# An attention, expert and MLP kernel on one core: two VectorE instructions swapped, a GpSimd step and sixteen transposes moved

## What is computed

```python
# 1. attention with a decaying complex state: B=4, H=8, S=768, D=48
mag = sqrt(a_re**2 + a_im**2); scale = minimum(mag, 0.999) / (mag + 1e-6)
for t in range(S):
    new_re = ar * S_re - ai * S_im          # ar, ai: a_re, a_im times scale at step t
    new_im = ar * S_im + ai * S_re
    S_re, S_im = new_re + outer(k[t], v[t]), new_im
    y[t] = q[t] @ S_re
# 2. x = y as 3072 rows of 384; each row goes to the one of 8 experts with the highest logit
h = relu(xe @ w1[e]); out[mask] = gate_w * (h @ w2[e])
# 3. h = (x @ m1) * (x @ m2) @ m3; result = h @ m_out
```

## Time and profile before

| | |
|---|---|
| median of 3 runs | 1012.51 us (1010.46 to 1018.81) |
| the profiled execution | 1015.03 us |
| its span, first to last instruction | 1013.3 us |
| TensorE busy | 924.8 us (91%) |
| VectorE busy | 439.8 us (43%) |
| ScalarE busy | 412.1 us (41%) |
| GpSimd busy | 394.7 us (39%) |
| mean granted TensorE clock | 0.980 |

### The profile page before, as it was taken

How to read it: one execution, slowest core, us unless ns; L and a number is a source line. 1 busy time by engine, 2 the same in 40 slices (tenths; PEclk the granted TensorE clock), 3 DMA queues, 4 the chain that set the end, 5 groups by cost and what they waited for, 6 DMA issues and landing times.

```text
span 1013.3 us, 17941 instructions
## 1 busy us (share of the span) xinstructions
PE 924.8 (91%) x6799; PEld 818.8 (81%) x6799; DVE 439.8 (43%) x703; ACT 412.1 (41%) x620; POOL 394.7 (39%) x230
## 2 busy tenths in 40 slices
PE   1678999889889699989999999998999999999996
PEld 1568888778878466979999999997898989898986
DVE  2559889979967360252222222222313131313130
ACT  4768798688654232232322322321222222222221
POOL 6336476676745342573373657610010101010101
PEclk9779999999999999999999999999999999999999
DMA  7714434534365147541532553411010101000000
GB/s 200 137 33 95 87 72 79 126 79 81 78 186 189 41 176 234 172 136 61 164 112 101 165 172 103 166 40 48 1 63 1 63 1 63 1 32 1 32 1 32
DMA packets 160151, 91.81 MB, mean 91 GB/s; under 512 B 128576, under 2 KB 152896, under 8 KB 160064
## 3 DMA queue, kind: packets, MB, share of 16 engines
q1 hardware_dynamic: 147344, 67.81, 25.1%
q10 hardware_dynamic: 9648, 13.30, 4.2%
q0 software_dynamic: 3072, 9.49, 2.4%
HBM read 71.77 MB, written 18.81 MB: 89 GB/s over the span
## 4 chain that ended last, share of the span: by engine, by line
PE 71%; DVE 15%; POOL 5%; issue 5%; ACT 2%; another core or an unknown queue 1%; DMA 0%; SPq 0%; ACTq 0%; DVEq 0%; POOLq 0%
PE psum L1840 19%; PE psum L1799 13%; PE psum L1777 12%; PE psum L1852 10%; PE psum L401 6%; PE psum L1686 4%; PE psum L1623 2%; DVE arena L1182 2%; DVE arena L1114 2%; DVE arena L1133 1%; PE psum L1649 1%; POOL x_by_expert L690 1%; DVE arena L1121 1%; POOL arena L671 1%; POOL arena L659 1%
## 5 line engine op out<-in xcount | busy, mean ns | idle before, releaser
L1840 PE MATMUL psum<-x2t,ring 128*128 128x512 f32 x864 | 197.1, 389 | 0.0
L1840 PEld LDWEIGHTS psum<-x2t,ring 128*128 128x128 f32 x864 | 162.1, 188 | 33.5
L401 PE MATMUL psum<-arena 128*128 128x128 f32 x925 | 130.3, 283 | 38.3 <-DVE arena L1114 21.9
L401 PEld LDWEIGHTS psum<-arena 128*128 128x128 f32 x925 | 110.2, 146 | 53.7 <-issue 42.8
L784 POOL DMA_INDIRECT out_dram<-arena x24 | 23.1, 963 | 320.9 <-ACT arena L1093 317.4
L1777 PE MATMUL psum<-ring,f_xt 128*128 x558 | 137.2, 400 | 4.4 <-DVE f_xt L1474 4.4
L1799 PE MATMUL psum<-ring,f_ht 128*128 x744 | 138.7, 341 | 2.0 <-DVE f_ht L1480 2.0
L1799 PEld LDWEIGHTS psum<-ring,f_ht 128*128 128x128 f32 x744 | 129.7, 190 | 2.4 <-issue 2.3
L1777 PEld LDWEIGHTS psum<-ring,f_xt 128*128 128x128 f32 x558 | 103.7, 190 | 26.0 <-issue 4.9
L1515 DVE TENSOR_TENSOR ab_f<-psum,a_sb 128x512 f32<-128x512 f32 x48 | 33.2, 692 | 204.6 <-ACT a_sb L1083 204.6
L1852 PE MATMUL psum<-wfold_half,ab 128*128 128x384 f32 x576 | 102.8, 336 | 0.0
(11 more groups left out here) (178 smaller groups left out, 1371.1 us busy)
## 6 DMA issues: line engine op xcount, KB each, us to landing
stage<-in_moe_w_dram SPq DMA_DIRECT2D x16, 1536.0 KB, 7.3
y_dense<-arena ACTq DMA_DIRECT2D x31, 194.0 KB, 2.7
arena<-x_by_expert ACTq DMA_DIRECT2D x28, 194.0 KB, 2.4
arena<-y_dense SPq DMA_DIRECT2D x24, 194.0 KB, 3.6
arena<-in_a_re_dram SPq DMA_DIRECT2D x24, 192.0 KB
arena<-in_a_im_dram SPq DMA_DIRECT2D x24, 192.0 KB
arena<-in_q_dram SPq DMA_DIRECT2D x24, 192.0 KB, 2.7
arena<-in_k_dram SPq DMA_DIRECT2D x24, 192.0 KB, 3.4
```

The lines of the kernel that those rows point to most:

```text
L401: return nc.tensor.transpose(psum[:, bank, c0:c0 + P], src, ident)
L1840: last = mm(psum[:, bank + j % 2, :], m_half[m][x][:, kc, j * P:(j + 1) * P], x2t[y][:, kc, :], start=(kc == 0 and x + y == 0), stop=(kc = ...
```

## The change

On VectorE, `clip(p)` goes ahead of `unit_check(p)`, and `ratio(p)` moves from ahead of the masks to behind the state. On GpSimd, `sum_angles` of a unit moves from the end of a unit's last step (i = 2, unit n + 2) into the next step (i = 0, unit n + 1), behind the three `root_prod` and ahead of the second half of the row sends and of `turn_q`. On TensorE and ScalarE, the transposes of fold blocks 2 and 3 and their copies move ahead of the last batch's ranks and exponential; the transposes now wait for the last masks, since they write the banks of the scores. Where the transposes stood, the count is followed by the first fold.

```diff
--- before.py
+++ after.py
@@ -698,7 +698,7 @@
 
             def step(k):
                 n, i = divmod(k, K)
-                p = n + 2
+                m, p = n + 1, n + 2
                 if i == 1 and k >= PICKED + 1 and (k - PICKED - 1) % C == 0:
                     tag_rows((k - PICKED - 1) // C)
                 if i == 2 and k >= PICKED + 2 and (k - PICKED - 2) % C == 0:
@@ -706,6 +706,8 @@
                 if i == 0 and 0 <= n < U:
                     for x in range(K):
                         root_prod(n, x)
+                if i == 0 and 0 <= m < U:
+                    sum_angles(m)
                 if i == 0 and k >= PICKED + 3 and (k - PICKED - 3) % C == 0:
                     scatter_rows((k - PICKED - 3) // C, K, C)
                 if 0 <= k < K * U:
@@ -714,8 +716,6 @@
                     add_squares(p)
                 if i == 1 and 0 < p < U:
                     ratio_seed(p)
-                if i == 2 and 0 <= p < U:
-                    sum_angles(p)
 
             add_squares(0)
             ratio_seed(0)
@@ -981,6 +981,8 @@
             for k in range(-4, K * U + 1):
                 step(k)
             rows_out(NT - 1)
+            fold_cols(EARLY, m3t_late)
+            fold_cols(EARLY + 1, m3t_late)
             exp_logits(B - 1)
             act.wait_ge(bad_ready, 1)
             with act.If(act.value_load(bad[0:1, 0:1], min_val=0, max_val=1) > 0):
@@ -998,9 +1000,8 @@
                     nc.scalar.activation(ex, lg, ACT.Exp).then_inc(g_exp, 1)
 
 
-            fold_cols(EARLY, m3t_late)
             for i in range(EARLY, NJ):
-                if i + 1 < NJ:
+                if EARLY < i < NJ - 1:
                     fold_cols(i + 1, m3t_late)
                 if i == EARLY:
                     act.wait_ge(y_done, K * U)
@@ -1303,8 +1304,6 @@
                         ends((a - 1) // K)
                 if i == 2 and k >= PICKED + 2 and (k - PICKED - 2) % C == 0:
                     weigh((k - PICKED - 2) // C)
-                if i == 2 and 0 < p < U:
-                    ratio(p)
                 if k == -1:
                     fold_cols(0, m3t_early)
                     fold_cols(1, m3t_early)
@@ -1312,6 +1311,8 @@
                     mask(k - 1)
                 if k >= 2 and (k - 2) % C < C - 1:
                     state(k - 2)
+                if i == 2 and 0 < p < U:
+                    ratio(p)
                 if 0 <= k < K * U:
                     weigh_inputs(n, i)
                     turn_k(n, i)
@@ -1322,8 +1323,8 @@
                 if i == 0 and k >= PICKED and (k - PICKED) % C == 0:
                     pick((k - PICKED) // C)
                 if i == 1 and 0 < p < U:
+                    clip(p)
                     unit_check(p)
-                    clip(p)
                 if i == 2 and 0 <= m < U:
                     inverse(m)
                 if k == 0:
@@ -1673,6 +1674,8 @@
                 for half in range(2):
                     if i:
                         pe.wait_ge(m3t_copied, 2 * i - 1 + half)
+                    if i == EARLY and half == 0:
+                        pe.wait_ge(att_masked, 2 * K * U)
                     for j in range(4):
                         last = tr(A_BANK + half, j * P, m3s[m3_buf(i)][:, (4 * half + j) * P:(4 * half + j + 1) * P])
                     last.then_inc(m3t_done, 1)
@@ -1722,6 +1725,8 @@
             for k in range(-4, K * U + 1):
                 step(k)
             rows_t(NT - 1)
+            fold_t(EARLY, m3_late)
+            fold_t(EARLY + 1, m3_late)
             rank_rows(B - 1, rank_done, hot_done)
             pe.wait_ge(bad_ready, 1)
             with pe.If(pe.value_load(bad[0:1, 0:1], min_val=0, max_val=1) > 0):
@@ -1744,11 +1749,10 @@
             mm(psum[:, RANK_BANK, COUNT_COL:COUNT_COL + E], ones, seen, start=True, stop=True).then_inc(count_done, 1)
 
             pe.wait_ge(x_done, NT)
-            fold_t(EARLY, m3_late)
-            for i in range(EARLY, NJ):
-                if i + 1 < NJ:
+            for i in range(EARLY, NJ - 1):
+                if i > EARLY:
                     fold_t(i + 1, m3_late)
-                    fold(i, m3t_late, mo_late)
+                fold(i, m3t_late, mo_late)
 
             pe.wait_ge(table_ready, 1)
```

## The result

| | before | changed |
|---|---|---|
| median | 1012.54 us (20 runs, 1008.92 to 1018.81) | 1015.86 us (20 runs, 1013.64 to 1017.92) |
| ratio, 95% interval | | 1.0035 [1.0023, 1.0047] |
| profiled execution | 1015.03 us, span 1013.3 | 1016.47 us, span 1014.8 |
| mean granted TensorE clock | 0.980 | 0.979 |

The changed kernel is 3.3 us slower. The forecast was 1014.7 us, range 1004 to 1019, within 1% at 0.88: it held. Several terms under it did not. The prediction took 10 us for the least that can be told of this kernel; twenty runs of each told 3.3. The profile of before lies 2.5 us above its median, the one of after 0.6 above its own, so their difference of 1.4 us is smaller than the 3.3 of the medians. I compare the traces step by step instead. A step is named by the chunk whose scores TensorE computes in it.

A forecast was written before the change was run, and what follows sets the result against it. TensorE, 71% of the chain, was taken to bound the kernel, with VectorE's chain to `turn_k` inside each unit. Terms 0.6 - 0.3 + 2.5 + 0.5 + 0.8 - 1.9 = +2.2 us gave a median of 1014.7, range 1004 to 1019.

The forecast's parts named there:

- The copy L1138 is held: VectorE's 12-element copy inside SBUF waits until GpSimd's L636 ends, about 2 us instead of 0.16.
- rival (a): The copy L1138 does not wait, so `turn_k` comes 1.4 us earlier in ordinary units; sum -6.1, 1006.4 us; chance 0.20.
- Clip, six units: VectorE's stall moves from L1114 to L1138, `turn_k` gains 0.06 us a unit; -0.3 us over six units, bounds -7 and 0.
- Prologue: Same edit for unit 1: L1138 waits, so the copies that let TensorE start the first fold start later; +0.6 us.
- step 0: Unit 1's two sums now stand between root products and `turn_q`; TensorE's wait grows from 2.95 to near 5.4; +2.5 us.
- nothing hides it: At the first step's `turn_q`, the reason for taking the upper of the bounds 0 and 2.5 us as the delay.
- Sums, ordinary units: `turn_q` comes 0.4 us later with 0.5 to spare; VectorE's 0.95 gained in the inverse lies beside TensorE's work; 0 us.
- the units in which the expert is picked: Two units bound by VectorE: the pick is still held by GpSimd's add of squares, 0.4 us later; +0.8 for two.
- Sums, units that send rows: Two units where TensorE waits for GpSimd's L671: 0.4 us later less 0.1 from earlier sends; +0.5 for two.
- Transposes: Tail: 16 transposes move into TensorE's idle time, 3.4 us gone, 1.6 lost to the first fold at half speed; -1.9 us.
- the upper bound: In the tail: +4.0 us if loads of blocks 6 and 7, about 8 us earlier, delay TensorE's code behind the branch.
- Rival (b): `turn_q` of a unit's first chunk, behind GpSimd between inverse and scores, bounds every unit; +4 on top, 1018.7 us; chance 0.12.

The follow-up runs named there:

- e4_ends_late: Changed kernel with the 12-column copy of the ends moved behind the state; 1003.87 us against 1009.52 for the kernel before, ratio 0.9938.
- e5_sum1_early: Changed kernel with unit 1's sums of angles back in the prologue; one run for its trace: step 0 scores 9.8 us after the inverse's start, 12.4 in the changed kernel.
- e2_sums: Kernel before with only the sums of angles moved; 1012.78 us against 1009.52, ratio 1.0036.
- e1_clip: Kernel before with only the clip ahead of the sum check and the ratio behind the state; 1009.63 us against 1009.52, ratio 0.9995.
- e10_best: Kernel before with clip first, ratio and copy of the ends behind the state, transposes moved, block 6 and 7 loads held until the count; 1004.09 us against 1013.63, 0.9898.
- e11_after_filler: Changed kernel with 24 constant transposes ahead of the scores of steps 12 and 18; 1013.71 us against 1013.63 for the kernel before, 0.9991; changed kernel beside it 1015.69.
- e8_sums_filler: Kernel before with only the sums moved, plus 24 constant transposes ahead of the scores of steps 12 and 18; 1012.84 us against 1008.0 for the kernel before, 1.0041.
- e3_transposes: Kernel before with only the transposes and their copies moved; 1009.34 us against 1009.52, ratio 0.9993.
- e6_loads_late: Changed kernel with SyncE holding the loads of m3 blocks 6 and 7 until the count; one run for its trace: the wait ahead of the count 3.38 us.
- e7_clip_ends: Kernel before with clip first, ratio and copy of the ends behind the state, sums and transposes as before; 1001.37 us against 1008.0, ratio 0.9938.

## Why the prediction was right, point by point

- **The copy L1138 is held: right.** 2.25 us beside L636, in eight places 1.98 in the mean. On the rule of the Trainium skill that the prediction cites, SBUF — State Buffer, "Who interferes with whom", the trace now agrees: the copy, second to issue, waited until GpSimd's instruction ended. This was the step on which "same" and not "faster" hung, and e4_ends_late shows it: with the copy elsewhere the gain of rival (a) is there. Rival (a) stood 8.3 us below the forecast (1006.4 for 1014.7); taking the copy away brought 6 to 10 us.
- **Clip, six units: -0.3 forecast.** In the unit shown it is -0.2 (10.04 to 9.82), near -1.3 if all six gain as much.
- **Prologue +0.6 and step 0 +2.5: together 3.1 forecast, +0.34 measured at step 1.** In the prologue the delay of the copies was right (L1212 starts 6.1 us after L1111, 5.6 before), but nothing of it is left at the inverse (22.8 us after L1111, 22.9 before). At step 0 the delay of the scores was right (12.4 for 9.85), the step "nothing hides it" failed, and the wait ahead of the scores, forecast near 5.4, is 0.28: TensorE had run these scores at half clock, and now the phases, waiting for the sums too, ran directly ahead of them and took the low clock on themselves. That the profile before had lost the clock there is chance (e5_sum1_early); in an execution that kept it, the step would have been right.
- **Sums, ordinary units: 0 forecast**, right at steps 6 and 21, **-0.93 measured** at step 3. There the inverse's shorter second half (2.71 to 1.76) lies on VectorE's chain to the next `turn_k`; I had put it beside TensorE's work. (L1149 fell to 1.76 in seven of its eight places, at the last it is 2.72.) In the units in which the expert is picked I forecast +0.4 each; they gained 0.93 and gave back 0.8.
- **Sums, units that send rows: +0.5 forecast, +5.4 measured.** This is the mis-sized term that makes the kernel slower, and e2_sums carries the whole loss. Steps 12 and 18 lose 1.46 and 1.16. Of that, the sums ahead of the sends and `turn_q` cost 0.6 each, twice what was counted. At step 12 another 0.87 comes from the first half of the inverse, held by L671; this is not the doing of the moved sums, since in e1_clip and e10_best, where they are in their old place, L671 held it too (it took 3.90 us, 1.05 later from inverse to scores). At step 18 the other 0.55 stands ahead of the inverse. Steps 13 and 19 then lose 1.25 and 1.51 to the clock, which I had put at nothing; e11_after_filler got about 2 of the two back, e8_sums_filler did not.
- **Transposes: -1.9 forecast, +0.6 between the two profiles, about -1 in the mean of six traces with and six without, nothing that the timing of e3_transposes can tell.** 3.4 us left, as counted. The first fold cost 2.8 more in place of 1.6, as it ran some 5.5 us at 0.50. And of the upper bound, a longer wait ahead of the count, some 1.2 us came true, which e6_loads_late took away again; that it is a wait for code remains a guess.

The sum of the terms by these traces is 0.3 - 1.3 - 0.9 - 0.3 + 5.4 + 0.6 = +3.8 against +2.96 found at block 4; the rest of -0.8 lies mostly between step 23 and `rows_t`. That the forecast's +2.2 came near the +3.3 of the medians is luck in the sizes: a loss of 5 us that I did not see stood against gains that I did not see, and against delays that were hidden. The mechanism of the clip was right; the one that makes the kernel slower, the clock behind the sends, is not in the prediction. Rival (b) had the place right, GpSimd between inverse and scores, and at step 12 also its condition, an inverse held by another GpSimd instruction. It did not come true in the ordinary units (12.8 us from inverse to scores at step 6, as before), and its 4 us came near only because the clock, which it did not name, made up for that.

What stays open: why a wait of 2.04 us lost the clock in one trace and 2.81 kept it in another; why e8_sums_filler kept the clock and brought no time; whether the sums still cost anything beside the late copy; what TensorE waits for ahead of the count; and which part of e10_best's gain over e7_clip_ends is real.

## What to carry to other kernels

When two instructions are swapped so that one no longer meets another engine's long SBUF operation, look for the next SBUF-to-SBUF instruction in the order, however small: it takes over the whole wait; moving a 12-column copy was worth 6 to 10 us here. Price a longer wait of TensorE twice, once for the wait and once for the work behind it at half clock, and look at the same place in several executions, since one that kept the clock may lose it in the next. Where transfers start earlier because a buffer comes free earlier, check what is fetched at that moment, and hold them back if nobody needs them.

## What the runs showed of the hardware

- A copy of 12 columns is held about as long as an instruction on 1152 columns: 0.16 us alone, 2.25 beside a running GpSimd instruction with two SBUF operands (2.1 more; L1114, on 1152 columns, took 3.67 for 1.36, 2.3 more). L1143, which reads PSUM and one SBUF operand, kept its 0.68 us at that instruction's start.
- Two waits of 4.27 and 3.40 us cost 1.25 and 1.51 us more behind them, through scores of 3.30 and 3.58 us at a granted clock of 0.50 to 0.75. Waits of 1.78 (e4_ends_late, step 18: scores of 3.20 us) and 2.04 us lost the clock too, one of 2.81 kept it. Transposes of a constant in the wait kept it at 1.00; one pair of kernels returned 2.0 us of device time by them, another nothing.
- The loads of two m3 blocks, started some 9 us earlier (counted from `rows_t`), lengthened a wait that no instruction ends from 2.7 to 3.6 us (eight traces without them) to 4.0 to 4.9 (six with them).
